# Tile 0's attention in eight PSUM banks, its weights scaled by GpSimd, and the first two q tiles loaded through ScalarE's queue

## What is computed

```python
kv_pool = kv.reshape(B, H // r, r, W // r, r, C).mean(axis=(2, 4))      # r = 4
k = v = kv_pool.reshape(B, -1, C) @ w_sr                                # 768 keys, C = 128
s = (q @ k.transpose(0, 2, 1)) / np.sqrt(C)
a = np.exp(s - s.max(-1, keepdims=True))
x = (a / (a.sum(-1, keepdims=True) + 1e-09)) @ v                        # 12288 tokens
h = x @ w_in1;  x = (h / (1 + np.exp(-1.702 * h))) @ w_out1             # 128 -> 2048 -> 128
h = x @ w_in2;  out = (h * np.clip(h + 3, 0, 6) / 6) @ w_out2
```

## Time and profile before

| | |
|---|---|
| median of 3 runs | 1311.92 us (1311.71 to 1314.39) |
| profiled execution | 1314.29 us, its span 1312.6 us |
| TensorE busy | 1277.8 us, 97% |
| VectorE busy | 1037.8 us, 79% |
| ScalarE busy | 1031.9 us, 79% |
| GpSimd busy | 36.1 us, 3% |

### The profile page before, as it was taken

One profiled execution on the slowest core, in us unless ns is written; L12 is line 12 of the kernel. 1 busy time (PEld: TensorE's weight loads), 2 busy tenths in 40 slices (PEclk: granted clock), 3 DMA queues, 4 the chain that ended last, 5 costly groups with the idle time before them and its releaser, 6 DMA issues.

```text
span 1312.6 us, 18302 instructions
## 1 busy us (share of the span) xinstructions
PE 1277.8 (97%) x5748; PEld 1061.8 (81%) x5748; DVE 1037.8 (79%) x1073; ACT 1031.9 (79%) x1211; POOL 36.1 (3%) x43
## 2 busy tenths in 40 slices
PE   6799999999999999999999999999999999999996
PEld 6578888888888888888888888888888888888775
DVE  4777788888888888788888887887887788888666
ACT  2678788788888888788888878878888788888665
POOL 1900000000000000000000000000000000000000
PEclk9999999999999999999999999999999999999999
DMA  8332203213023032131130320311302303203000
GB/s 269 91 73 53 64 9 72 48 24 72 22 50 72 0 72 48 24 72 31 41 72 5 67 58 14 72 41 31 72 15 57 66 6 72 48 16 65 9 0 17
DMA packets 186948, 65.94 MB, mean 50 GB/s; under 512 B 108720, under 2 KB 179504, under 8 KB 186672
## 3 DMA queue, kind: packets, MB, share of 16 engines
q1 hardware_dynamic: 186928, 65.69, 22.3%
HBM read 23.13 MB, written 6.34 MB: 22 GB/s over the span
## 4 chain that ended last, share of the span: by engine, by line
PE 94%; DVE 3%; ACT 2%; DMA 1%; issue 0%; SPq 0%; DVEq 0%; ACTq 0%
PE pair L791 16%; PE pair L793 15%; PE pair L792 15%; PE bank_av L791 9%; PE bank_av L792 9%; PE bank_av L793 9%; PE bank_out L791 7%; PE bank_out L792 6%; PE bank_out L793 6%; PE pair L805 1%; DMA kv_sb<-in_kv_dram 1%; DVE mid_lo L665 1%; DVE neg_max L599 0%; DVE work L658 0%; ACT work L446 0%
## 5 line engine op out<-in xcount | busy, mean ns | idle before, releaser
L665 DVE TENSOR_TENSOR mid_lo<-work,mid_hi 128x1024 fp32r<-128x1024 f32 (+1 forms) x193 | 234.9, 1218 | 135.4 <-ACT mid_hi L459 135.2
L791 PE MATMUL pair<-x_hi,w_hi 128*128 128x512 f32 x768 | 302.6, 394 | 6.0 <-DVE x_lo L641 3.7
L792 PE MATMUL pair<-x_lo,w_hi 128*128 128x512 f32 x768 | 299.7, 390 | 0.0
L793 PE MATMUL pair<-x_hi,w_lo 128*128 128x512 f32 x768 | 299.6, 390 | 0.0
L431 ACT ACTIVATE work<-pair 128x1024 f32<-128x1024 f32 x192 | 197.0, 1026 | 127.1 <-PE pair L793 124.9
L649 DVE TENSOR_TENSOR mid_lo<-work,mid_hi 128x1024 fp32r<-128x1024 f32 x192 | 235.8, 1229 | 32.4 <-ACT mid_hi L438 32.4
L658 DVE SCALAR_TENSOR_TENSOR work<-work,pair 128x1024 f32<-128x1024 f32 (+1 forms) x193 | 232.5, 1205 | 10.3 <-ACT work L446 10.2
L446 ACT ACTIVATE work<-pair,half 128x1024 f32<-128x1024 f32 (+1 forms) x193 | 212.1, 1099 | 12.4 <-PE pair L793 11.8
L438 ACT ACTIVATE mid_hi<-work 128x1024 fp32r<-128x1024 f32 x192 | 202.8, 1056 | 5.6 <-PE bank_av L793 3.4
L459 ACT ACTIVATE mid_hi<-work 128x1024 fp32r<-128x1024 f32 (+1 forms) x193 | 201.5, 1044 | 0.5 <-DVE work L658 0.5
L791 PEld LDWEIGHTS pair<-x_hi,w_hi 128*128 128x128 f32 x768 | 144.5, 188 | 44.8 <-ACT work L431 7.1
(11 more groups left out here) (87 smaller groups left out, 1506.3 us busy)
## 6 DMA issues: line engine op xcount, KB each, us to landing
p_keys<-p_turned SPq DMA_DIRECT2D x368, 96.0 KB, 2.2
inv_b<-inv_dram SPq DMA_DIRECT2D x24, 256.0 KB, 3.3
q_raw<-in_q_dram SPq DMA_DIRECT2D x92, 64.0 KB, 2.0
out_dram<-y_sb SPq DMA_DIRECT2D x92, 64.0 KB, 2.4
kv_sb<-in_kv_dram SPq DMA_DIRECT2D x7, 768.0 KB, 11.1
w_raw<-in_moe_w_in_dram SPq DMA_DIRECT2D x2, 1024.0 KB, 8.0
inv_dram<-inv_t SPq DMA_DIRECT2D x96, 0.5 KB
kv_sb<-in_kv_dram SPq DMA_DIRECT2D x3, 256.0 KB, 11.5
```

The lines of the kernel that those rows point to most:

```text
L665: dve.tensor_tensor(mid_lo[mid2(t, p)][:, part], act2[p % 2][:, part], mid_hi[mid2(t, p)][:, part], ALU.subtract).then_inc(mid2_ready, 1)
L791: pe.matmul(dst, a_hi, b_hi, start=start, stop=False)
L792: pe.matmul(dst, a_hi, b_lo, start=False, stop=False)
L793: return pe.matmul(dst, a_lo, b_hi, start=False, stop=stop)
```

## The change

For tile 0, and for the q of tiles 0 and 1:

- ScalarE's queue issues q of tile 0 (one load), w_sr and q of tile 1 (four loads), in pieces of 512 bytes; SP starts with kv, whose last two groups now come by rows. The q tiles are transposed by TensorE, at the head of its list, into bank_out and bank_av; VectorE's list starts with both `q_low_first`.
- The key copies of parts 1 and 2 make k_hi straight from PSUM first, and k_full afterwards. The second half of the values is turned in bank_out.
- The four slots of tile 0 have their scores in pair[0], pair[1], pair[2] and `both_banks` (bank_av with bank_out), so all eight banks. When a slot's exponential is done, VectorE forms its inverse (`inverse_first`), GpSimd multiplies the slot's weights by it in place, ahead of the weight split, TensorE turns the slot with six transposes (`turn_probs`) into the banks that its scores had, and `p_hi_first` and `p_lo_first` take 768 columns.
- The values are weighed by halves of the tile (`weigh_first`: slots 0 and 1, then 2 and 3), 18 matmuls of 256 columns each, into pair[0]; `x1_high_first` and `x1_low_first` read the output there. No inverse of tile 0 goes through DRAM, and `scale_x(0)` is gone.
- The scores of tile 1 stand between the two halves. Its `turn_p` all come ahead of the FFN of tile 0, two of them ahead of `x1_low_first(1)`.

The core of the diff, with renumbered semaphores left out:

```diff
+    q_first = q[:, 0:TILE].rearrange("b (s p) c -> p (b s) c", p=128)
+    q_second = q[:, TILE:2 * TILE].rearrange("b (a s i) c -> i (b a) s c", a=4, i=32)
...
-                return pair[(0, 1, 2, 0)[s]]
+                return (pair[0], pair[1], pair[2], both_banks)[s]
             if isinstance(u, int) and u == 1:
-                return pair[(1, 0, 1, 0)[s]]
+                return (pair[2], pair[1], both_banks, pair[2])[s]
...
-            return pair[0] if isinstance(t, int) and t == 0 and p % 2 else pair[2]
+            return pair[1 - p % 2] if isinstance(t, int) and t == 0 else pair[2]
...
+            turned = halves(scores_in(0, s)).rearrange("p h (j n) -> p h j n", n=128)
...
+            chunks = p[:, :].rearrange("p (h j n) -> p h j n", h=2, n=TILE)[:, :, :, s * 128:(s + 1) * 128]
...
+            return pair[0][:, h * 512:h * 512 + TILE // 2]
...
+        VALUES_IN = [pair[2][:, 0:HALF], bank_out[:, 0:HALF]]
...
-            sp.dma_start(w_sr_sb[:, :], w_sr).then_inc(w_sr_loaded, 16)
...
-                if g < KV_GROUPS - 1:
+                if g < KV_GROUPS - ROW_GROUPS:
...
-            load_q(0, q_raw, q_loaded)
-            load_q(1, q_raw1, q1_loaded)
...
-            sp.wait_ge(qt_ready, 1)
+
+            load_weights(0, w_in1)
+            load_weights(1, wo_view[0])
+            load_weights(2, w_in2)
+            load_weights(3, wo_view[1])
+            sp.wait_ge(qt_first_ready, 1)
             load_q(2, q_raw, q_loaded)
...
-            spread_inv(0)
             spread_p(1)
             spread_inv(1)
...
+            for s in range(SLOTS):
+
+                hold(first_inv_ready, s + 1)
+                pool.tensor_scalar(slot(probs_first, s), slot(probs_first, s), p_inv[:, s:s + 1], None,
+                                   ALU.mult).then_inc(first_normed, 1)
...
+            def q_high_first(u):
+                act.wait_ge(qt_first_ready, u + 1)
+                act.activation((q_hi, q1_hi)[u][:, :], (bank_out, bank_av)[u][:, :], ACT.Copy,
+                               scale=SCALE).then_inc(q_hi_ready, 1)
...
+                if s == 0 and isinstance(u, int) and u == 1:
+                    act.wait_ge(first_sum_ready, SLOTS)
...
+            def p_hi_first(s, h=None):
+                act.wait_ge(pt_ready, s + 1 + (h or 0))
+                act.activation(first_in_chunks(p_high, s, h), turned_in(s, h), ACT.Copy).then_inc(pt_hi_ready, 1)
...
+            def x1_high_first(h):
+                act.wait_ge((av_half_done, av_done)[h], 1)
+                act.activation(x1_hi[:, of_tile(h)], first_output(h),
+                               ACT.Copy).then_inc((x1_half_hi_ready, x1_hi_ready)[h], 1)
...
+            act.dma_start(q_raw[:, :].rearrange("p (s c) -> p s c", s=SLOTS), q_first).then_inc(q0_loaded, 16)
+            act.dma_start(w_sr_sb[:, :], w_sr).then_inc(w_sr_loaded, 16)
+            for a in range(4):
+                act.dma_start(q_raw1[32 * a:32 * (a + 1), :].rearrange("p (s c) -> p s c", s=SLOTS),
+                              q_second[:, a]).then_inc(q1_loaded, 16)
+
+            q_high_first(0)
+            q_high_first(1)
             pooled_copy(0)
             k_copies(0)
             v_hi_copy(0)
             pooled_copy(1)
+            k_hi_copy(1)
             pooled_copy(2)
-            q_high(0)
-            k_copies(1)
-            k_copies_last()
+            k_hi_copy(2)
+            k_full_copy(1)
+            k_full_copy(2)
             v_hi_copy(1)
             for s in range(SLOTS):
                 exponential(0, s)
-                if s == 0:
-                    q_high(1)
-            exponential(1, 0)
-            for k in range(KC):
-                p_hi_first(k)
-                if k % 2 == 1:
-                    exponential(1, 1 + k // 2)
-            x1_high(0)
+            for s in range(SLOTS - 1):
+                p_hi_first(s)
+            for h in range(2):
+                p_hi_first(SLOTS - 1, h)
+            x1_high_first(0)
+            for s in range(SLOTS):
+                exponential(1, s)
+            x1_high_first(1)
             load_table(ACT.Gelu_apprx_sigmoid)
...
+            def q_low_first(u):
+                dve.wait_ge(q_hi_ready, u + 1)
+                dve.scalar_tensor_tensor(out=(q_lo, q1_lo)[u][:, :], in0=(bank_out, bank_av)[u][:, :], scalar=SCALE,
+                                         in1=(q_hi, q1_hi)[u][:, :], op0=ALU.mult,
+                                         op1=ALU.subtract).then_inc(q_lo_ready, 1)
...
+            def inverse_first(s):
+                part = slice(s, s + 1)
+                dve.wait_ge(exp_ready, s + 1)
+                dve.tensor_scalar(p_sum_eps[:, part], p_sum[:, part], 1e-9, None,
+                                  ALU.add).then_inc(first_sum_ready, 1)
+                dve.wait_ge(first_sum_ready, s + 1)
+                dve.reciprocal(p_inv[:, part], p_sum_eps[:, part]).then_inc(first_inv_ready, 1)
...
+            def x1_low_first(h):
+                dve.wait_ge((x1_half_hi_ready, x1_hi_ready)[h], 1)
+                last = dve.tensor_tensor(x1_lo[:, of_tile(h)], first_output(h), x1_hi[:, of_tile(h)], ALU.subtract)
+                if h == 1:
+                    last.then_inc(x1_ready, 1)
...
-            for g in range(6):
+            q_low_first(0)
+            q_low_first(1)
+            for g in range(KV_GROUPS - ROW_GROUPS):
                 add_pixels(g)
             k_lo_part(0)
-            add_pixels(6)
             for a in range(KV_ROWS):
-                add_row_pixels(a)
-                if a == 0:
-                    v_lo_part(0)
-            turn_q(0)
-            q_low(0)
+                add_row_pixels(KV_GROUPS - 2, a)
+            v_lo_part(0)
+            for a in range(KV_ROWS):
+                add_row_pixels(KV_GROUPS - 1, a)
             k_lo_part(1)
             k_lo_part(2)
+            maximum(0, 0)
+            v_lo_part(1)
+            maximum(0, 1)
+            maximum(0, 2)
+            inverse_first(0)
+            maximum(0, 3)
+            for s in range(1, SLOTS):
+                inverse_first(s)
+            for s in range(SLOTS - 1):
+                p_lo_first(s)
+            for h in range(2):
+                p_lo_first(SLOTS - 1, h)
+            x1_low_first(0)
             for s in range(SLOTS):
-                maximum(0, s)
-                if s == 0:
-                    v_lo_part(1)
-                    turn_q(1)
-                if s == 2:
-                    q_low(1)
-            maximum(1, 0)
-            inverse(0)
-            for k in range(KC):
-                p_lo_first(k)
-                if k % 2 == 1:
-                    maximum(1, 1 + k // 2)
-            scale_x(0)
-            inverse(1)
-            x1_low(0)
+                maximum(1, s)
             turn_p(1, 0)
             turn_p(1, 1)
+            x1_low_first(1)
+            turn_p(1, 2)
+            turn_p(1, 3)
+            inverse(1)
 
             for p in range(PAIRS):
                 act1_lo(0, p)
-                if p in (0, 1):
-                    turn_p(1, 2 + p)
...
+            def turn_q_first(u):
+                if u == 0:
+                    pe.wait_ge(q0_loaded, 16)
+                else:
+                    pe.wait_ge(q1_loaded, 16 * 4)
+                for s in range(SLOTS):
+                    last = pe.transpose((bank_out, bank_av)[u][:, s * 128:(s + 1) * 128],
+                                        (q_raw, q_raw1)[u][:, s * 128:(s + 1) * 128], ident[:, :])
+                last.then_inc(qt_first_ready, 1)
...
+            def turn_probs(s):
+                pe.wait_ge(first_normed, s + 1)
+                for k in range(KC):
+                    last = pe.transpose(turned_in(s)[:, k // 3, k % 3],
                                         slot(probs_first, s)[:, k * 128:(k + 1) * 128], ident[:, :])
-                last.then_inc(pt_ready, 1)
+                    if k == KC - 1 or s == SLOTS - 1 and k == KC // 2 - 1:
+                        last.then_inc(pt_ready, 1)
...
+            def weigh_first(h):
+
+                pe.wait_ge(pt_lo_ready, 2 if h == 0 else SLOTS)
+                for k in range(KC):
+                    if h == 1 and k == KC // 2:
+                        pe.wait_ge(pt_lo_ready, SLOTS + 1)
+                    cols = slice(k * 128, (k + 1) * 128)
+                    moving = slice(k * TILE + of_tile(h).start, k * TILE + of_tile(h).stop)
+                    last = product(first_output(h), v_hi[:, cols], v_lo[:, cols], p_high[:, moving],
+                                   p_low[:, moving], k == 0, k == KC - 1)
+                last.then_inc((av_half_done, av_done)[h], 1)
...
+            turn_q_first(0)
+            turn_q_first(1)
             for g in range(5):
                 pool_group(g)
             pe.wait_ge(w_sr_loaded, 16)
             keys_of(0)
             pool_group(5)
             values_of(0)
-            pool_group(6)
-            pool_group(7)
+            for a in range(KV_ROWS):
```

(66 more changed lines are left out.)

145 lines of the change are left out of this document (55 added, 90 removed).

## The result

The changed kernel took 1324.7 us (1323.19 to 1326.44, median of 6 runs), the kernel before 1312.45 beside it: a ratio of 1.009, interval 1.0079 to 1.01. I had forecast 1308.2 and at most 1312.5. The profiled run took 1324.24 us, its span 1322.5, which is 9.9 over the span before. On the medians the loss is 12.3, since the profiled run of the kernel before (1314.29) lay above its median.

A forecast was written before the change was run, and what follows sets the result against it. TensorE bounds the kernel, so only an earlier start of its dense work could gain: 3.4 + 1.2 + 0.5 - 0.9 - 0.5 = 3.7 us, giving 1310.6 profiled, 1308.2 as a median. The range ran from 1305.5 to 1312.5.

The forecast's parts named there:

- What bounds the kernel: Whole kernel: TensorE is busy 97% of the span; only an earlier start of its dense work can win time.
- Loading: Opening: q of tile 1 lands at 6.5, slot 0 is scored at 28.6 instead of 29.6; gain 1.0 (bounds -1.5 and 2).
- kv 1.2 us later: Loading: q issued beside kv delays kv by 1.2 us from the second group on (bounds 0 and 2.5).
- The 0.87 us of waiting for q_low: End of loading: TensorE's wait at 27.75 goes since q is ready long before; part of the gain of 1.0.
- GpSimd's scaling: Attention of tile 0: multiplying a slot's 768 columns by the inverse column takes 0.93 us, with 1.93 the dearer reading.
- The clock in the transposes: Rival, chance 0.20: between slot 3's scores and weigh_first(0) transposes lose TensorE's clock; gain only 0.4, profile time 1311.5.
- late q: Rival, chance 0.12: q of tile 1 lands at 13.3, five groups end at 26.8; 3.3 slower than now, 1315.2.
- lost clock: Rival, chance 0.20: TensorE's clock falls during tile 0's transposes, which become the pace, and weighing starts at half speed; 1311.5.
- dear scaling: Rival, chance 0.08: GpSimd's scaling takes 1.93 a slot in tile 0's attention, the four end 4 us later; 1312.2.
- The clock did not hold in the way I said: Entry into the FFN: the gap of 2.2 us is too short for the clock to fall; gain 1.2 (bounds 0 and 1.2).
- Attention as a whole: Tile 0, first maximum to FFN: x1 ready at 48.7 against 52.1; gain 3.4, the 1.0 of loading included.
- The split's toll: FFN of tile 0: GpSimd's later weight split slows VectorE; last projection waits 0.9 more, stalls and p_low of tile 1 0.5.

The follow-up runs named there:

- repaired: Changed kernel with q of tile 1 loaded behind group 6's rows, VectorE scaling by the column, x1_low_first(1) ahead of both turn_p, GpSimd's split held after two pieces: 1310.67 us.
- late_q1: Changed kernel with the same loads, but q of tile 1 transposed, copied and subtracted later in the engines' lists: 1320.55 us against 1313.58 before.
- q1_behind: Changed kernel with q of tile 1 loaded by SP behind the rows of group 6 and transposed behind those rows: 1317.56 us against 1312.94 before.
- repaired_nohold: Same as repaired, but GpSimd's weight split is not held and runs from when the weights land: 1311.17 us against 1312.94 before.
- late_q1_imm: late_q1 with GpSimd multiplying by constants 1.0 instead of the inverse column, leaving tile 0 unnormalised: 1313.44 us against 1313.58 before.
- late_q1_fill: late_q1 plus matmuls with overwritten output where TensorE waits for GpSimd (34 behind the last scores, 14 behind each of three slots): 1319.29 us against 1312.94 before.
- q1_2k: Changed kernel with q of tile 1 in one load of 128 pieces of 2 KB instead of four loads of 512-byte pieces: 1321.68 us against 1310.98 before.

## Why the prediction was wrong, step by step

- **What bounds the kernel** was right: the loss, as the gain of repaired, is in the time at which the dense work starts.
- **Loading: the step that failed.** "q of tile 1 I take as landed at 6.5": it landed at 14.0. I took it from w_sr's 1.9 us, a load alone ahead of all others, for one that shares the engines with kv. The rival was nearly exact: a landing at 13.3 and five groups pooled by 26.8, against 14.0 and 27.2. It put the first maximum 7 us behind the forecast's 28.6, and it came 7.5 behind. What failed was the choice between the two, on one row of a load that had the queue to itself. The lateness became a loss because both lists put q ahead of kv, which late_q1 shows.
- **kv 1.2 us later** (bounds 0 and 2.5) was 2.2 at the sixth add of late_q1, inside the bounds. But I had it begin at the second group; 1.75 of it was there at the first.
- **The 0.87 us of waiting for q_low** did go: from k_lo(0) to the first maximum q1_behind takes 7.2 us, before 7.9. But its k_lo(0) is 0.7 later, where the forecast had it 0.2 later and the time behind it at 6.7. So the gain of 1.0 came out as 0.1; repaired and repaired_nohold have 0.2 and 0.8.
- **GpSimd's scaling: the second step that failed.** I took 0.93 "since it is the same operation with one tensor". With constants that was right (0.83). A column operand made it 2.19, above even the bound of 1.93. Rows 9 held no row with such an operand, and the choice of the lower end had only that likeness behind it.
- **The clock in the transposes** fell as the rival had it, with a cost in the weighing near its 1.3 (1.8), but for another reason: its condition was that transposes don't hold the clock, and late_q1_imm and repaired show that they can hold it and bring it back. What stood around them was idling, here that of the slow scaling; in repaired, with 1.2 and 0.9 us of it, the clock fell too.
- **Adding up:** I gave late q, lost clock and dear scaling 0.12, 0.20 and 0.08 as if they excluded each other, and all three came. Their prices on the forecast were 7.0, 3.3 and 4.0; 1308.2 and these make 1322.5, and 1324.7 was measured. That is close by luck. 2.0 of the 3.3 was for transposes that set the pace, which late_q1_fill shows to be worth nothing beside GpSimd's 2.19; and the 4.0 was a slip, since four slots at 1.93 back to back from 32.4 end at 40.1, 3.2 behind the forecast's 36.9. The markers close the sum: 7.5 late at the first maximum, 4.4 more from there to the weighing (13.6 against 9.2) and 2.2 more from there to the FFN (13.2 against 11.0), together 14.1. On 1310.6, the forecast for a profiled run, that makes 1324.7, and the profiled run took 1324.24. The dear scaling brings the lost clock with it, so those two were hardly separate cases at all.
- **Right in size**: 256 columns step by 0.12; two turn_p and a subtraction make 2.2 to 2.3 of gap; from the FFN's start to the first projection 5.9 was forecast and 5.8 measured, against 7.1 before. The clock did not hold in the way I said, though: it fell 1.4 us into the FFN (a stretch 65:66 at 0.50). Behind the same gap of 2.3 us it fell in five of the eight kernels that have it, between 0.1 us ahead of the FFN and 1.4 into it, and held in late_q1_imm, late_q1_fill and q1_2k; the runs don't say what decides. Where it fell the first projection came after 5.8 to 6.6 us, where it held after 5.1 to 5.6. So the 5.9 was met with the clock lost, which is luck.
- **Attention as a whole**: from the first maximum to the FFN I had 20.2 us. late_q1_imm has 19.7, repaired 19.4, the changed kernel 26.9, before 22.6. So the reordering gains what I said once the scaling is cheap.
- **The split's toll** was about right as a sum: from the FFN's start to tile 2 it is 29.7 us before, 29.3 by the forecast, 29.3 in the changed kernel and 29.6 in late_q1_imm (28.9 to 30.3 in all eight kernels with that order). The place was another: VectorE's three p_low of tile 1, beside a split that ends at 89.5, take 5.00 us in place of 3.49. That it is a toll is borne out by repaired_nohold, where the split ends at 66: the three take 3.49, and from the FFN's start to tile 2 it is 27.5.
- **What then keeps late_q1_imm level**, where the forecast, with cheap scaling and early q, had 3.7 us of gain: its first maximum is 2.1 late, where I had it 1.0 early. That is 3.1 us, and 2.8 are missing at tile 2: the attention gave 0.5 more than forecast, the rest 0.2 less. kv is the larger part of the 2.1. Some 0.8 is not: in late_q1, with the sixth add at 20.69 against 20.82 here, the first maximum is only 1.2 late, and what differs is TensorE's pooling, 6.59 us for 36 matmuls against 7.49 here. The granted clock is 1.00 in both, and why the pace differs the traces don't show.

## What to carry to other kernels

A load that a second queue issues beside a full first one is not early because its list is; put the wait for it where the first queue's own data would be waited for anyway. An operation with a per-partition column is not the same operation as with a constant: unless a row shows it on that engine, keep the dear bound. And rivals that can happen together must be added up before the range is drawn.

## What the runs showed of the hardware

- GpSimd: a multiply of 768 float32 columns takes 0.81 to 0.83 us with constants, 2.19 with a column. VectorE does the one with a column in 0.62, and mostly in 0.97 to 1.49 where GpSimd's weight split runs beside it.
- Two DMA queues: beside SP's queue ScalarE's got about 15% of the engines' time as a mean from 6 to 11 us, with pieces of 512 bytes and of 2 KB alike; 256 KB landed 9.6 to 12.2 us after the first issue.
- The clock stayed at 1.00 between scores and weighing where TensorE idled 1.6 us ahead of the transposes and 0.22 between the first slots (late_q1_imm). It fell with 1.2 us ahead and 0.9 between (repaired), and with 3 and 1.3 (changed). In repaired it came back 3.4 us later, at 38.7, behind nothing but transposes; in the changed kernel, where TensorE ran 1.54 us of transposes in every 2.19, it stayed at 1.2 GHz from 43.9 until 4.3 us into the weighing.
